# Moving the weight splits and two loads within the start of a fused attention and MLP kernel

## What is computed

```python
# q, k, v: (8, 8, 576, 64); x: (4608, 512); d_ff = 1536
kv  = einsum('bhsd,bhse->bhde', k, v)
out = einsum('bhsd,bhde->bhse', q, kv)
rms = sqrt(mean(out * out, axis=-1) + 1e-06)
x   = (out / rms * g_norm), heads side by side        # (4608, 512)
x   = (sigmoid(x @ w_gate) * (x @ w_val)) @ w_out     # first MLP
x   = (silu(x @ w2_gate) * (x @ w2_val)) @ w2_out     # second MLP
```

## Time and profile before

| | |
|---|---|
| median of 3 runs | 1813.48 us (1812.95 to 1816.47) |
| profiled execution | 1815.67 us |
| its span in the profile | 1813.9 us |
| PE busy | 1751.3 us, 97% |
| DVE, ACT, POOL busy | 1209.0, 896.5, 370.9 us |
| DMA | 366.93 MB, mean 202 GB/s |

### The profile page before, as it was taken

How to read it: one execution, slowest core, us unless ns; L and a number is a source line. 1 busy time by engine, 2 the same in 40 slices (tenths; PEclk the granted TensorE clock), 3 DMA queues, 4 the chain that set the end, 5 groups by cost and what they waited for, 6 DMA issues and landing times.

```text
span 1813.9 us, 30783 instructions
## 1 busy us (share of the span) xinstructions
PE 1751.3 (97%) x11210; PEld 1700.2 (94%) x11210; DVE 1209.0 (67%) x1898; ACT 896.5 (49%) x1687; POOL 370.9 (20%) x326
## 2 busy tenths in 40 slices
PE   7899999999999999999999899998999999999998
PEld 5789999998999999999998899998999999999997
DVE  3666776777656678666669777776765568655554
ACT  3656666555444445444445555555444445444444
POOL 4622221013111124111144000004211124111111
PEclk9799999999999999999999999999999999999999
DMA  8688878465665566565555555565655666455542
GB/s 197 178 251 251 250 216 267 181 238 187 213 202 205 200 227 231 206 207 205 204 166 190 192 192 192 192 217 189 221 199 205 204 225 230 141 187 188 188 179 78
DMA packets 199831, 366.93 MB, mean 202 GB/s; under 512 B 49664, under 2 KB 159744, under 8 KB 199680
## 3 DMA queue, kind: packets, MB, share of 16 engines
q1 hardware_dynamic: 199680, 364.96, 60.2%
HBM read 234.36 MB, written 130.55 MB: 201 GB/s over the span
## 4 chain that ended last, share of the span: by engine, by line
PE 72%; issue 10%; DVE 6%; POOL 4%; DMA 4%; SPq 2%; ACT 1%; POOLq 0%; DVEq 0%; ACTq 0%
PE ps L695 67%; PE ps L598 2%; DMA wops<-in_moe_w_gate_dram 1%; POOL arena L1341 1%; PE ps L583 1%; DVE xo L1029 1%; PE ps L637 1%; DMA arena<-x 1%; POOL rrms L1294 1%; PE ps L588 1%; DVE arena L1146 1%; DVE hop L1103 1%; SPq L410 1%; POOL wops L1304 1%; POOL wops L1302 1%
## 5 line engine op out<-in xcount | busy, mean ns | idle before, releaser
L695 PE MATMUL ps<-xo,wa 128*128 128x384 f32 x6048 | 1086.9, 337 | 16.1 <-ACT arena L867 10.7
L695 PEld LDWEIGHTS ps<-xo,wa 128*128 128x128 f32 x6048 | 1049.4, 188 | 23.6 <-ACT arena L867 13.1
L1146 DVE TENSOR_TENSOR arena<-ps,arena 128x384 f32<-128x384 f32 x648 | 351.5, 553 | 374.2 <-PE ps L695 296.3
L867 ACT ACTIVATE arena<-ps 128x384 f32<-128x384 f32 x648 | 317.6, 491 | 572.8 <-PE ps L695 572.0
L695 PE MATMUL ps<-hop,wb 128*128 128x384 f32 x3024 | 544.6, 337 | 17.0 <-DVE arena L1164 7.1
L695 PEld LDWEIGHTS ps<-hop,wb 128*128 128x128 f32 x3024 | 524.4, 188 | 26.9 <-DVE arena L1146 8.9
L1103 DVE TENSOR_TENSOR hop<-arena,hop 128x384 fp32r<-128x384 f32 (+1 forms) x396 | 288.2, 750 | 42.0 <-ACT hop L849 35.8
L1341 POOL TENSOR_TENSOR arena<-arena 128x384 f32<-128x384 f32 x144 | 145.6, 1033 | 761.7 <-DVE arena L1146 761.7
L849 ACT ACTIVATE hop<-arena 128x384 fp32r<-128x384 f32 (+1 forms) x396 | 233.3, 609 | 72.0 <-DVE arena L1164 39.0
L881 ACT ACTIVATE arena<-arena 128x384 f32<-128x384 f32 x216 | 112.6, 521 | 67.3 <-DVE arena L1146 67.2
L1164 DVE TENSOR_TENSOR arena<-arena 128x384 f32<-128x384 f32 x216 | 127.7, 593 | 20.4 <-DVE arena L1146 0.9
(11 more groups left out here) (67 smaller groups left out, 822.3 us busy)
## 6 DMA issues: line engine op xcount, KB each, us to landing
xo<-x_operands SPq DMA_DIRECT2D x168, 768.0 KB, 6.3
x_operands<-xo SPq DMA_DIRECT2D x84, 768.0 KB, 4.6
x<-arena SPq DMA_DIRECT2D x120, 384.0 KB, 3.2
arena<-x SPq DMA_DIRECT2D x96, 384.0 KB, 4.2
xraw<-x SPq DMA_DIRECT2D x22, 768.0 KB, 7.1
out_dram<-wops SPq DMA_DIRECT2D x48, 192.0 KB, 2.1
wops<-in_moe_w_gate_dram SPq DMA_DIRECT2D x24, 256.0 KB, 5.1
wops<-in_moe_w_val_dram SPq DMA_DIRECT2D x24, 256.0 KB, 5.9
```

The costliest lines, as they stand in the source:

```text
L695: mm = pe.matmul(dst, lhsT, rhs, start=(pr in (1, 5, 2) and c == 0 and i == 0), stop=(c == 1 and i == 2), skip_group_check=(pr in (6, 7, 4 ...
L867: nc.scalar.activation(dst, X(side), ACT.Copy).then_inc(copied, 1)
L1146: nc.vector.tensor_tensor(dst, acc, buf, ALU.add).then_inc(summed, 1)
```

## The change

Four things are moved; no arithmetic is added or dropped.

1. SP issues the loads of unit 7 directly behind those of unit 6 and ahead of weight unit 3, those of units 9 and 10 each ahead of a store or a weight load.
2. Weight units 0 to 3 are split in steps 3, 5, 6 and 8 (before: 4, 5, 6, 7), and weight unit 4 in window g == 0 (before: step 9). Both x splits are in step 7 (before: 7 and 8).
3. DVE's order in a step was scaling, sums, splits. It is now scaling, splits, sums. In step 8, PE and ACT take the output of unit 7 ahead of k^T v and q^T of unit 8, and DVE scales unit 7 behind the sums of unit 8.
4. In window g == 0 PE does six entries (before: two) ahead of x^T of unit 7. ACT and DVE take the splits of weight units 4 and 5 in later places, and POOL takes weight unit 5's differences behind the inverse root of unit 9 (before: ahead of it).

```diff
-        W_STEP = {4: 0, 5: 1, 6: 2, 7: 3, 9: 4}
-        X_STEP = {7: 1, 8: 2}
+        W_STEP = {3: 0, 5: 1, 6: 2, 8: 3}
+        X_STEP = 7
-        KVQ_0, O_0, XT_0 = {3: 9, 12: 10, 20: 11}, {7: 9, 16: 10, 24: 11}, {1: 7, 11: 8, 19: 9, 27: 10}
+        KVQ_0, O_0, XT_0 = {5: 9, 12: 10, 20: 11}, {7: 9, 16: 10, 24: 11}, {5: 7, 11: 8, 19: 9, 27: 10}
...
             load_unit(6)
+            load_unit(7)
             load_w(3)
-            load_unit(7)
+            load_unit(8)
             store_xT(4)
-            load_unit(8)
             load_w(4)
+            load_unit(9)
             store_xT(5)
-            load_unit(9)
+            load_unit(10)
             load_w(5)
-            load_unit(10)
             store_xT(6)
... PE, the ten steps (ACT has the same with unit_sq)
-                if t <= SHARED:
+                if t < SHARED:
                     unit_kv_qT(t)
                 if t >= 1:
                     unit_o(t - 1)
+                if t == SHARED:
+                    unit_kv_qT(t)
... ACT, the ten steps, and window g == 0
-                if t in X_STEP:
-                    split_x(0, X_STEP[t])
+                if t == X_STEP:
+                    split_x(0, 1)
+                    split_x(0, 2)
...
+                        copy(1, 0)
+                        copy(1, 1)
                         unit_xT(7)
+                        unit_kv_qT(9)
                         split_x(0, 5)
-                        copy(1, 0)
                         split_x(0, 6)
-                        copy(1, 1)
-                        unit_kv_qT(9)
+                        unit_sq(9)
                         gated(11)
-                        unit_sq(9)
-                        split_w(5)
+                        split_w(4)
+                        unit_xT(8)
                         split_x(0, 7)
                         split_x(0, 4)
-                        unit_xT(8)
+                        split_w(5)
                         split_x(0, 3)
                         copy(6, 0)
... DVE, the ten steps, and window g == 0
-                if t >= 2:
+                if 2 <= t <= SHARED:
                     unit_scale(t - 2)
+                if t in W_STEP:
+                    split_w(W_STEP[t])
+                if t == X_STEP:
+                    split_x(0, 1)
+                    split_x(0, 2)
                 if t >= 1:
                     unit_norm(t - 1)
-                if t in W_STEP:
-                    split_w(W_STEP[t])
-                if t in X_STEP:
-                    split_x(0, X_STEP[t])
+            unit_scale(SHARED - 1)
...
                         x_s1_s3(0)
                         split_x(0, 5)
-                        unit_scale(8)
                         x_s2(0)
                         split_x(0, 6)
                         total(11, 0)
                         total(11, 1)
+                        unit_scale(8)
                         unit_norm(9)
                         hidden(11)
-                        split_w(5)
+                        split_w(4)
                         x_s4(0)
                         split_x(0, 7)
                         split_x(0, 4)
                         unit_scale(9)
+                        split_w(5)
                         split_x(0, 3)
... POOL
             rsqrt(8)
+            differences(4)
+            rsqrt(9)
             differences(5)
-            rsqrt(9)
```

More of the change, by code:

```diff
@@ L702, in _ @@
                         if g == 0:
+                            if at in XT_0:
+                                unit_xT(XT_0[at])
                             if at in KVQ_0:
@@ L706, in _ @@
                                 unit_o(O_0[at])
-                            if at in XT_0:
-                                unit_xT(XT_0[at])
                             continue
```

## The result

The changed kernel takes 1826.03 us (median of 4 runs, 1825.32 to 1826.56) beside 1813.22 of before (4 runs, 1811.69 to 1816.47): ratio 1.0068, 95% interval 1.0051 to 1.0085, so 0.5 to 0.85% slower. The forecast was + 8 us; measured are + 12.8 between the medians and + 9.9 between the two profiled executions (1825.56 and 1815.67).

The account below looks back on a forecast made before the run. PE, busy 97% of the span, was taken as the bound, so only the start could change. Removed stops were outweighed by delayed sums and half clock; weight unit 5's split came 8.1 us later: 1813.5 + 8 = 1821.5, range 1811 to 1828.

Parts of the forecast that it names:

- The loads: Start of kernel: weight unit 0 split earlier, unit 6's load out 5 us earlier; PE's 5.17 us stop goes.
- The order in a step: Steps: sums wait for the splits; squares to x^T takes 8.9 us (7.7 with x splits) in place of 5.4.
- The clock: Steps: PE idling about 4 us brings half clock; a step takes 7.8 us instead of 4.3, first one taken as 6.1.
- my three cases: Clock in the steps: mixed (taken), full throughout, half throughout; outputs of unit 8 end at 66.9, 60.0 or 68.6 us.
- Window g == 0: After the steps: x^T of unit 7 at 72.1 us (before 66.34), split of weight unit 5 ends 20.1 us later.
- split 5: End of DVE's split of weight unit 5, in window g == 0: forecast at 92.2 us instead of 84.1.
- Unit 12: Behind the window: load lands 19.6 us after weight unit 5's split, 8.1 us later than before; PE stops 3 to 5 us.
- The sum: Whole kernel: + 8 us on the median of 1813.5, giving 1821.5; 1818 to 1825 given chance 0.5.
- the lower bound: Range from the clock cases: full clock in every step, x^T of unit 7 at 65.9 us, + 2 us in all.
- the much slower case: Half clock from 31 us through window g == 0 and again before unit 12: + 13.5 us, 1827; chance 0.15.
- The faster case: Clock stays full in units 3 to 7, stops of 5.17 and 3.41 us won: 1807.5 us; chance 0.15.
- the one without a measurable change: All steps at full clock, or unit 12's load less bound to weight unit 5's split: + 2 us, 1815.5; chance 0.2.

Follow-up runs that it names:

- e3: Kernel before with only SyncE's new order of loads (unit 7 ahead of weight unit 3, units 8 to 10 as changed): ratio 1.0023 to the kernel before.
- e1: Kernel before with one edit, VectorE doing scaling, splits, sums instead of scaling, sums, splits: ratio 1.0020, 1818.21 us beside 1814.91.
- e2: Changed kernel with one edit, VectorE doing the sums ahead of the splits again: ratio 1.0014 to the kernel before, against 1.0068 of the whole change.
- f2: Changed kernel with filler matmuls ahead of x^T in steps 5, 7 and 8 (four, four, one): ratio 1.0043 to the kernel before.
- f1: Changed kernel with POOL taking weight unit 5's differences ahead of the inverse root of unit 9 again: ratio 1.0069 to the kernel before.
- g1: Changed kernel with only SyncE's stores of x operands 5, 6, 7 and 4 moved ahead of the load of unit 11: ratio 1.0040 to the kernel before.
- f4: Kernel before with the stores of x operands 5 and 6 moved ahead of the load of unit 11: ratio 0.9986 to the kernel before.
- g4: New loads and weight-split steps, sums first, old window, weight unit 4 in step 9, stores 5 and 6 early, fillers in steps 5, 7, 8, 9: ratio 0.9970.
- f3: Changed kernel with sums ahead of splits, weight unit 5's differences ahead of unit 9's root, four x stores ahead of unit 11's load: ratio 0.9968, 1810.56 us.

## Why the prediction came out as it did

- **The loads.** Right: no stop at unit 6, its load out at 29.84. That moving unit 7's load costs nothing held in the changed kernel, but for a narrower reason than I gave: e3 shows that the new order of loads costs 0.23% where weight unit 3 keeps its step.
- **The order in a step.** Right, and the main term. The forecast times were 33.0, 48.0 and 63.5 for x^T of units 2, 4 and 6; measured 33.27, 48.09 and 63.72. e1 (adding it alone, + 0.20%) and e2 (removing it alone, - 0.54%) show it as the cause from both sides. The saving on the roots is real (2.27 at 51.11 instead of 3.99) and far too small. That it hangs on who starts first is seen in e3: the root at 31.44 came 0.16 us behind a DVE split that had started at 31.28 and took 3.98 us. By the rule of the Trainium skill on the shared ports (page "SBUF — State Buffer", section "SBUF: two separate sides") it had to wait that split out, and the trace agrees: 31.28 + 2.02 + 2.27 is 35.6, and it ended at 35.4. The other way round the trace does not bear that rule out. POOL of the kernel before:

```profile
31.56 2.27 POOL L1294 TENSOR_TENSOR rrms<-msq,mhalf 96x12 f32<-96x12 f32 x1
```

  This root started 0.13 us ahead of the DVE split at 31.69; both ran side by side and took their usual 2.27 and 2.02 us.
- **The clock.** Right in kind: f2 puts its share of the loss at 3.4 us (mark) to 4.5 us (ratio). The mix I took (one step half and half, then half clock) matched this execution, and that the three times agree within 0.3 us is in part luck: in f1 the same steps came as with half clock throughout, the last of my three cases (40.8, 49.7 and 65.2 for x^T of units 3, 4 and 6; 40.53, 49.54 and 65.17 in f1).
- **Window g == 0.** x^T of unit 7 at 72.00 (forecast 72.1). The term that was mis-sized is the stretch from there (T) to the end of split 5: forecast 20.1, measured 22.6. 1.0 us of the difference arises ahead of POOL's differences: DVE's first two x combinations took 2.8 us instead of 1.9, beside the differences of weight unit 4, so that the root of unit 9 ended at T + 13.6 and not T + 12.6. Another 1.4 us are the differences of weight unit 5 themselves, 5.2 us beside DVE where I took 3.8. DVE's own operations of that time stretched too (2.55, 1.48 and twice 1.45 us instead of 2.02, 0.95 and twice 0.95); its list, which I put at T + 16, ended at T + 19.6. It still hid behind POOL and ACT, by 0.95 us, and f1 shows it as the next limit.
- **Unit 12.** Right: it landed 19.4 us behind its trigger (forecast 19.6). That the way runs through the stores is shown by g1. The stop itself was 2.1 and 0.3 us, not 3 to 5. The lowered clock behind it, which I had kept out of the sum, came in part: 3.50 instead of 2.35 us for twelve matmuls.
- **The sum.** 8.1 us forecast at split 5, 10.5 measured; with about 1.2 us for the clock that makes 11.6 at the mark. The time, 1826.0, lies within the range but near its upper end, and above the 1818 to 1825 to which I gave 0.5. In the lower bound, 60.0 + 3.9 + 2, the 3.9 has no row; my own price of the 18 matmuls at full clock is 3.5. And the waits at full clock between 20 and 30 us, 0.3 us in the rows, reach 0.89 us in the trace (at 27.34).
- **The rivals.** The median lies 1 us from the 1827 of the much slower case, to which I gave 0.15, but not by its way: in the profiled execution the clock was full again in part of 30 to 50 us and in nearly all of 70 to 80, and it fell once more near 90 and at unit 12. The faster case and the one without a measurable change did not come.

The parts do not add up: alone or removed they give 9.8 (order), 4.5 (fillers), 4.5 (window) and 5.0 us (stores) of 12.3, each uncertain by some 4 us. Their sum is 23.8, since they overlap: taking out the order also takes out idle time that the fillers fill, and the stores and the clock cost something in the kernel before as well (f4 gains 2.5 us there).

## What to carry to other kernels

Before moving a long operation ahead of a short one in an engine's list, ask whose chain the short one feeds: here a reduction of 0.95 us fed the inverse root, the scaling and PE, and standing behind a split that itself waits for ACT cost more than a removed DMA stop of 5.2 us gave. When a stop is taken away, look at once for the load that is released by the same work further on; here it was enough to issue the stores ahead of that load and not behind it. Where a short chain must idle PE, dummy matmuls ahead of the awaited one kept the clock (f2, g4), but they paid only where PE, and not the other engines, was then the last.

## What was not expected of the hardware

- The contention between DVE and POOL goes both ways: POOL's difference of 0.72 us took 2.04 us when it started beside a DVE split (e3 at 49.16), and DVE's operations of 0.95 us with SBUF operands took 1.3 to 1.5 us beside POOL's differences (f1 at 79.32 and 81.70). It depends on the order of the starts: the root at 31.56 in the kernel before, ahead of a split, lengthened nothing.
- Filler matmuls alone moved the time by about 0.25%, with every data dependence unchanged: 4.5 us in a kernel of 1826 us (3.4 at the mark), from 30 us of full clock, where the stretches had 0.66, 0.85 and 0.50.
- A busy PE did not mean a full clock: with its small attention matmuls it was busy for all of 50 to 60 us in the changed kernel and all of 30 to 50 us in f3, and the granted clock was 0.50 in both.
